# The last expert slot of a mixture-of-experts kernel as a branch of its own on TensorE

## The reference, cut to what matters

```python
for b in range(B):
    prev_e = -1
    for s in range(S):
        fresh_e = int(np.argmax(logits[b, s]))
        if s == 0 or local_gate[b, s] < 0.5:
            e = fresh_e
        else:
            e = prev_e if prev_e >= 0 else fresh_e
        prev_e = e
        ...
        h = np.maximum(x[b, s] @ w1[e], 0.0)
        out[b, s] = p[e] * (h @ w2[e])
```

## Time and profile before

| what | value |
|---|---|
| median of the runs | 385.42 us (384.82 to 387.62) |
| the profiled execution | 384.97 us, span 383.1 us |
| TensorE busy | 372.5 us (97% of the span) |
| VectorE, ScalarE, GpSimd busy | 75%, 41%, 36% |
| slots in use (outputs scaled at L1964) | 14, so slot 13 is the last |
| last matmul ends | 376.4 us |

### The profile page before, as it was taken

The page is one execution under the profiler, slowest core; times in us unless marked ns, Lnnn a source line. Parts: engine busy times, 40 slices in busy tenths (PEclk is TensorE's granted clock), DMA queues, the critical chain, the costliest instruction groups (busy, mean ns, idle before and its releaser), DMA issues.

```text
span 383.1 us, 8871 instructions
## 1 busy us (share of the span) xinstructions
PE 372.5 (97%) x3056; PEld 338.6 (88%) x3056; DVE 285.5 (75%) x630; ACT 155.4 (41%) x281; POOL 137.5 (36%) x114
## 2 busy tenths in 40 slices
PE   8999999999999999999999999999999999999993
PEld 6899999999999999999999656789999999999982
DVE  7799899988897997868878568798546764647440
ACT  6556313212322221241441254368525852555530
POOL 2999784911760570100004006303332233223231
PEclk9999999999999999999999999999999999999998
DMA  7999603302500330500038484799874287111011
GB/s 218 328 329 285 212 22 113 112 21 67 157 36 21 110 110 26 181 3 22 21 97 286 134 308 144 264 372 305 301 277 151 87 277 284 43 34 43 26 45 43
DMA packets 32923, 56.67 MB, mean 148 GB/s; under 512 B 3294, under 2 KB 20484, under 8 KB 32753
## 3 DMA queue, kind: packets, MB, share of 16 engines
q1 hardware_dynamic: 30576, 49.84, 39.9%
q0 software_dynamic: 2304, 6.30, 5.3%
HBM read 51.41 MB, written 5.51 MB: 149 GB/s over the span
## 4 chain that ended last, share of the span: by engine, by line
PE 91%; DVE 5%; issue 1%; DMA 1%; ACT 1%; POOL 0%; SPq 0%; POOLq 0%; DVEq 0%; ACTq 0%
PE bank L1039 18%; PE bank L935 7%; PE bank L937 7%; PE bank L936 7%; PE bank L1367 5%; PE bank L1339 5%; PE bank L1375 5%; PE bank L1371 5%; PE bank L1343 5%; PE bank L1346 5%; PE bank L1356 3%; PE bank L953 3%; PE bank L1268 3%; PE bank L1245 3%; PE bank L984 2%; PE bank L974 2%
## 5 line engine op out<-in xcount | busy, mean ns | idle before, releaser
L1039 PE MATMUL bank<-xnT_hi,parts 128*128 128x256 f32 x432 | 65.3, 287 | 0.5 <-ACT xnT_hi L726 0.2
L1677 DVE SCALAR_TENSOR_TENSOR stage<-stage 128x384 f32<-128x384 f32 x81 | 60.7, 791 | 0.1
L1039 PEld LDWEIGHTS bank<-xnT_hi,parts 128*128 128x128 f32 x432 | 56.6, 191 | 2.0 <-ACT xnT_hi L726 0.5
L733 ACT ACTIVATE parts<-bank 128x512 fp32r<-128x512 f32 x36 | 21.5, 597 | 90.6 <-PE bank L1039 90.5
L667 POOL DMA_INDIRECT out_y<-late x14 | 20.5, 1462 | 93.9 <-DVE late L1964 93.9
L935 PE MATMUL bank<-parts 128*128 128x384 f32 x144 | 49.3, 342 | 0.0
L937 PE MATMUL bank<-parts 128*128 128x384 f32 x144 | 48.2, 335 | 0.0
L936 PE MATMUL bank<-parts 128*128 128x384 f32 x144 | 48.2, 334 | 0.0
L813 ACT ACTIVATE parts<-stage (+1 forms) x32 | 46.2, 1485 | 0.4 <-DMA stage<-in_w 0.4
L1933 DVE TENSOR_TENSOR parts<-stage,parts x24 | 41.1, 1755 | 4.9 <-ACT parts L813 4.2
L1039 PE MATMUL bank<-xnT_lo,parts 128*128 128x256 f32 x216 | 37.4, 282 | 0.0
(11 more groups left out here) (257 smaller groups left out, 732.6 us busy)
## 6 DMA issues: line engine op xcount, KB each, us to landing
stage<-in_w SPq DMA_DIRECT2D x36, 768.0 KB, 6.7
stage<-in_w_ch SPq DMA_DIRECT2D x6, 768.0 KB, 7.8
arena<-in_k_t SPq DMA_DIRECT2D x12, 224.0 KB, 3.2
arena<-in_r_t SPq DMA_DIRECT2D x12, 224.0 KB, 3.1
arena<-in_v_rows SPq DMA_DIRECT2D x12, 192.0 KB, 3.9
arena<-in_k_rows SPq DMA_DIRECT2D x12, 192.0 KB, 3.2
x_rows<-stage SPq DMA_DIRECT2D x12, 192.0 KB, 1.9
arena<-in_r_rows SPq DMA_DIRECT2D x10, 192.0 KB, 3.3
```

The source lines that it names most:

```text
L733: act.activation(hT_hi[:, 2 * q:2 * q + 2, :].rearrange("p a t -> p (a t)"), bk[6 + q % 2][:], ACT.Relu).then_inc(h_hi_ready, 1)
L1039: mm = pe.matmul(acc, w[:, k, at], x[:, k, :], start=start and k == 0, stop=stop and k == KD - 1, skip_group_check=first and q == 0)
L1677: dve.scalar_tensor_tensor(spent[n % NSPENT], x2[t % 2], 1.0, wgr[e], ALU.mult, ALU.mult, accum_out=lg[:, t, e:e + 1]).then_inc(s_spent, 1)
```

## The change: what it does

TensorE's stream alone is written by another function, `live_slots_apart`. The flag of the next slot is still read once for each slot from slot 9 on, but before the slot, and a slot is now there twice: once with its work ahead and everything that follows (under `live > 0`, no further condition inside), and once without it (under `live < 1`). The last slot in use is always the second kind. Since the following slots are nested in the first branch, the second kind of slot s stands behind the code of all the slots from s to 17.

```diff
+        def live_slots_apart(eng, body, s=0):
+
+            if s + 1 < LIVE:
+                body(s, None)
+                live_slots_apart(eng, body, s + 1)
+            elif s + 1 == NSLOT:
+                body(s, False)
+            else:
+                live = eng.value_load(slot_tab[0:1, 1, s + 1:s + 2], min_val=0, max_val=1)
+                with eng.If(live > 0):
+                    body(s, None)
+                    live_slots_apart(eng, body, s + 1)
+                with eng.If(live < 1):
+                    body(s, False)
+
...
             hidden_e(0, 0, 1)
             pe.wait_ge(rt_v, RT_TABLES)
-            live_slots(pe, slot)
+            live_slots_apart(pe, slot)
```

## The result

The changed kernel takes **388.89 us** (median of 11 runs, 387.62 to 390.75) against 386.31 us for the kernel before, timed beside it (11 runs, 384.82 to 387.62). The ratio is 1.0067, with a 95% interval of 1.0049 to 1.0085: 0.7% slower, by about 2.6 us. The profiled execution took 388.08 us, span 386.3 us; its counterpart before took 384.97 us, span 383.1 us.

A forecast was written before the change was run, and what follows sets the result against it. TensorE, busy for 97% of the span, was taken to bound the kernel. 384.97 us plus 3.0 us from the jump made 388.0 us, and 0.45 us more to the runs' median made 388.4 us; range 386.8 to 391.0 us.

The forecast's parts named there:

- What bounds the kernel: Whole span: TensorE is busy for 97% of it, its strip full until the last slice.
- the conditions at no price: Slots 9 to 12: removing their conditions gains 0, hidden by TensorE's full queue; 0.56 us at most without that cover.
- The jump: L391 to the last slot's part: taken at 368.5 us for 3.58 us, making the transposes' weights 3.0 us later.
- the loop's jump back: Lower end for L391's price: the loop's backward jump over its already run body costs 0.24 us.
- The room for 2048 instructions: First rival, at L391: if filled ahead, the jump finds its target and the time is 385.4 us; chance 10%.
- Behind the jump: Last slot, transposes to scatter: no other work fills in, so all 3.0 us reach the end.
- the second L386: Last slot: this 0.22 us branch goes but gives nothing, since it ran beside ScalarE's L904.
- the wait for ScalarE: Last slot, after 0.9 us of transposes: TensorE waits 1.1 us for ScalarE.
- The clock: Second rival, last slot: TensorE's clock falls in the new gap, giving 389.4 to 392.8 us, likeliest 390.5; chance 14%.
- The end: End of TensorE's stream: hidden under GpSimd's drain, which ends at 385.8 us, with 3.2 us to spare.
- The end jump: Slot 13 to the end, over 268 rows: costs 3.58 us at 374.6 us, harms nobody, and disappears with the change.
- The four skips at the end: Four L394 over 37 rows each: 0.9 to 1.4 us, hidden; as third rival setting the time, 389 to 392 us, 3%.

The follow-up runs named there:

- e4: The change with TensorE's stream written out for 15 slots instead of 18, the jump over 103 rows instead of 421; 384.32 us in one run.
- e8: The change with TensorE's stream written out for 16 slots instead of 18, the jump over 210 rows instead of 421; 387.98 us in one run.
- e1: The change with a slot's two branches swapped on TensorE, the last slot's part standing first; 384.05 us, ratio 0.9968 to the kernel before.
- e2: e1 plus a wait of TensorE's sequencer for VectorE's scaling of the last slot before it jumps to the end; 384.47 us, ratio 0.9971.
- e7: The kernel before with the number of slots set to the 14 in use, on all engines; 384.31 us, ratio 0.9947.
- e3: The change plus ten matmuls of zeros between the last slot's transposes and its output; 391.98 us, ratio 1.0164 to the kernel before.
- e9: e1 plus five idle reads by TensorE's sequencer ahead of the last slot's transposes; 388.48 us, ratio 1.0056 to the kernel before.
- e10: The change run once more, unaltered, for its profile; 387.92 us in one run.
- e5: The change plus four matmuls of zeros between the last slot's transposes and its output; 388.46 us, ratio 1.006 to the kernel before.
- e6: The change with the last-slot question asked before the preceding slot's output matmuls, which stand in both branches; 387.20 us, ratio 1.0022 to the kernel before.

## Why the prediction was right, and where it was not

**What bounds the kernel, and the conditions at no price: right.** A middle slot takes 9.56 us in both kernels. What was taken out was covered by the queue.

**The jump: right in place, price and effect.** L391 at 368.6 us (forecast 368.5), 3.44 us (3.58), the weights of the last transposes at 373.07 us (373.1), TensorE idle for 2.53 us (2.8). The nearest row, a forward jump into code not run before, was the right one to take, and the loop's jump back the wrong one. e4 and e8 show why: over 103 rows the target was there, over 210 it had to be fetched, as over 268 and 421. Two rules of the Trainium skill, "Runtime: NRT & Kernel Launch", section "Instruction fetch mechanics", stood against each other. The one that a taken branch to a target outside the current window must wait for its block agrees with the traces (one q8 packet in each of the 19 branches over 1 us). The room for 2048 instructions on TensorE didn't help L391, whose target hadn't been fetched.

**Behind the jump: 0.4 us off.** I let all 3.0 us reach the end; the output began 2.6 us later. In part that is where I measured. Before, the weights of the first transpose load 0.33 us ahead of the end of slot 12's matmuls (370.09 and 370.42 us), and with the change TensorE starts right behind its weights; so weights that load 3.0 us later make transposes that begin 2.7 us later (373.10 against 370.42 us). The rest is in the stretch from there to the output, 1.54 us before and 1.47 us after, and 1.27 us in e1, e2 and e4, where no pause comes first. It isn't the second L386 that was saved, since e7's last slot has none either and takes 1.53 us. What differs is the time from the end of ScalarE's first L904 (L919 with the change) to the first output matmul: 0.46 us before and in e7, where register steps of L1366 and L1367 lie in it, and 0.20 us with the change. I had also put the wait for ScalarE at 1.1 us; of the 1.54 us TensorE is busy for 0.88, so 0.66 us are idle.

**The clock: the term that was left out.** I gave it 14% as a rival, and as a mechanism it came: 24 matmuls in 5.98 us rather than 4.46, +1.5 us in the profiled execution, within the 1 to 3 us that I had named. Six profiled executions have a pause of 2.2 to 2.9 us ahead of the last slot's transposes, and the clock fell in five of them (the change, e3, e8, e9, e10) and not in e5. It fell in none without such a pause, nor in e6 with 1.6 us. It fell before the transposes in e3 (373.2 us), within them in e8 and e10, and behind them in the change and e9. My argument against it was that neither pause alone was as long as the one before the fall at the end, nearly 4 us. That was a single trace: behind the last matmul, where TensorE does nothing more, the clock fell after 2.2 us in e4 and after 5.2 us in e2, and somewhere between in the other eleven. A pause of 2.2 to 2.9 us thus lies at the lower end of what was enough, and whether one of them brings the clock down can't be told from its length.

**The end: a gain that I didn't see.** The end jump that disappears seems to have had a price after all: its fetch lay in the time of the last scatter, and with it went 1.0 us between the two profiled executions. The traces bear this out in order, but no run shows the cause by itself; in e1 the end jump stays, its fetch ends 1.8 us ahead of the scatter's packets, and the landing takes 2.5 us. I had costed that jump at nothing since TensorE's own end was hidden, and didn't ask what its fetch collides with on the DMA side.

The last two partly cancel (+1.5 and -1.0 us), so the 3.0 us of the jump alone came out close to the 3.1 us between the profiled executions and the 2.6 us between the medians. That is in part luck: of three terms the sum had one. The 388.4 us also rest on a median of 385.42 us from three runs, where eleven gave 386.31 us. The base was 0.9 us too low and the step 0.4 us too large, which leaves the 0.5 us to the measured 388.89 us. The four skips at the end behaved as forecast (0.35, 0.23 and 0.22 us, and one of 2.65 us that had to wait for a fetch, as I had allowed for) and stayed under GpSimd's drain.

## What to carry to other kernels

Where the engine's queue was full, conditions cost nothing here, and what counted of a branch was whether its target had been fetched. The path that is taken once, at the end, where nothing can fill in, should fall through; the far jump belongs behind the last dispatch. Before moving a jump, read the longest duration of each branch line in the trace, and compare it with the lead that the sequencer has on its engine at the new place.

## What the runs showed of the hardware

- A taken forward jump on TensorE's sequencer cost 0.2 to 0.5 us, or 1.8 to 4.3 us with one 16 KB packet on q8 in its time, the branch ending 1.3 to 1.5 us behind the packet. Over 103 rows of the list it was 0.35 us, over 210 rows 3.73 us, over 421 rows 3.44 us; the longest, 4.28 us, was at the end of e1. Of the four jumps over 37 rows at the end of the change, one cost 2.65 us.
- TensorE's sequencer was 2.6 us ahead of the engine behind matmuls of 384 columns (the change, 368.0 against 370.57 us), and 3.3 us behind those of 512 (e6). Of the sequencer's steps and stalls the engine lost what exceeded that: 2.53 us in the change, 1.60 us in e6.
- Ten small matmuls added to each last-slot part, of which four stand ahead of the one that runs, came with a wait of 1.1 us and another q8 packet within the transposes (e3). With four matmuls in each there was none (e5).
- In or up to 1.5 us behind pauses of 2.2 to 2.9 us TensorE fell to 1.2 GHz, for 3.4 us in four traces (the change, e8, e9, e10) and for 6.8 us in one (e3), and stayed at 2.4 GHz in one (e5). At the end of the program it fell 2.2 (e4) to 5.2 us (e2) after the last matmul.
- The last scatter was seen landed 2.5 us after its start where no instruction packet of q8 ended within 1 us ahead of its first packet, 2.8 to 2.9 us where one did, and 3.1 to 3.5 us where one ended among its packets (thirteen traces).
